# Attention and expert layers in one kernel: other places for two query loads, products of zeros ahead of the keys, another order of the value loads and means, and a ReLU in halves

## The reference

```python
# attention: a window of 16 either way, and 24 block summaries for all
k_sum = k.reshape(B, H, 24, 32, D).max(axis=3)
v_sum = v.reshape(B, H, 24, 32, D).mean(axis=3)
a = softmax([where(|i-j| < 16, scale*q@k.T, -1e9), scale*q@k_sum.T + log(32)])
attn = a @ concat([v, v_sum])
# first layer
h = x @ w_in
y = where(h > 0, h, exp(min(h, 0)) - 1) @ w_out
# second layer: the best expert of each token, times its gate
e = argmax(norm(y) @ norm(expert_emb).T / tau)
out = gate * (relu(y @ w1[e]) @ w2[e])
```

## Time and profile before

| what | value |
|---|---|
| median of 3 runs | 552.57 us (551.87 to 552.78) |
| the profiled execution's own time | 555.51 us |
| its span, first to last instruction | 553.8 us |
| TensorE busy, share of the span | 533.6 us, 96% |
| VectorE, ScalarE, GpSimd busy | 303.0, 234.3, 78.3 us |
| mean granted clock of TensorE | 0.992 of full |
| moved by DMA | 49.23 MB |

### The profile page before, as it was taken

How to read it: one execution, slowest core, us unless ns; L and a number is a source line. 1 busy time by engine, 2 the same in 40 slices (tenths; PEclk the granted TensorE clock), 3 DMA queues, 4 the chain that set the end, 5 groups by cost and what they waited for, 6 DMA issues and landing times.

```text
span 553.8 us, 11727 instructions
## 1 busy us (share of the span) xinstructions
PE 533.6 (96%) x3892; PEld 457.5 (83%) x3893; DVE 303.0 (55%) x672; ACT 234.3 (42%) x528; POOL 78.3 (14%) x210
## 2 busy tenths in 40 slices
PE   5898999999999999999999999999999999999995
PEld 4686888888888888888888899888778888888883
DVE  4667887544644465446642557667585265232552
ACT  5575664454544444444433245463072152121440
POOL 6300111010120000000000000110311222111221
PEclk9898999999999999999999999999999999999999
DMA  9999321323131112110100440010775156101000
GB/s 196 267 259 314 82 47 25 88 57 80 43 101 25 25 25 63 25 24 15 39 1 1 162 181 1 20 58 1 243 295 201 38 190 192 45 30 35 19 19 24
DMA packets 63499, 49.23 MB, mean 89 GB/s; under 512 B 46038, under 2 KB 52182, under 8 KB 63456
## 3 DMA queue, kind: packets, MB, share of 16 engines
q1 hardware_dynamic: 61056, 42.36, 26.7%
q0 software_dynamic: 2400, 6.30, 3.6%
HBM read 43.40 MB, written 6.82 MB: 91 GB/s over the span
## 4 chain that ended last, share of the span: by engine, by line
PE 93%; DVE 2%; DMA 2%; ACT 1%; issue 1%; SPq 1%; POOLq 0%; DVEq 0%; ACTq 0%
PE bank L932 24%; PE bank L974 8%; PE bank L981 8%; PE bank L987 8%; PE bank L1129 5%; PE bank L1171 5%; PE bank L1179 5%; PE bank L1137 5%; PE bank L1131 5%; PE bank L1173 5%; PE bank L910 2%; PE bank L892 2%; PE bank L1163 2%; PE bank L883 2%; DMA q_raw<-in_q 1%; PE bank L833 1%
## 5 line engine op out<-in xcount | busy, mean ns | idle before, releaser
L1324 ACT ACTIVATE el<-bank 128x512 f32<-128x512 f32 x48 | 28.7, 597 | 111.3 <-PE bank L932 110.0
L1605 DVE TENSOR_SCALAR el<-el 128x512 f32<-128x512 f32 x48 | 20.5, 427 | 90.2 <-ACT el L1324 90.2
L932 PE MATMUL bank<-x_hi,w_hi_parts 128*128 128x256 f32 x376 | 60.9, 283 | 0.0
L932 PE MATMUL bank<-x_hi,w_lo_parts 128*128 128x256 f32 x376 | 60.4, 282 | 0.0
L932 PE MATMUL bank<-x_lo,w_hi_parts 128*128 128x256 f32 x376 | 60.2, 282 | 0.0
L932 PEld LDWEIGHTS bank<-x_hi,w_hi_parts 128*128 128x128 f32 x376 | 53.6, 188 | 3.2 <-issue 0.2
L974 PE MATMUL bank<-w_hi_parts,g_hi 128*128 128x512 f32 x192 | 55.8, 413 | 0.0
L981 PE MATMUL bank<-w_lo_parts,g_hi 128*128 128x512 f32 x192 | 53.0, 398 | 0.0
L987 PE MATMUL bank<-w_hi_parts,g_lo 128*128 128x512 f32 x192 | 52.5, 395 | 0.0
L932 PEld LDWEIGHTS bank<-x_lo,w_hi_parts 128*128 128x128 f32 x376 | 51.5, 189 | 0.0
L932 PEld LDWEIGHTS bank<-x_hi,w_lo_parts 128*128 128x128 f32 x376 | 51.3, 188 | 0.0
(11 more groups left out here) (268 smaller groups left out, 909.5 us busy)
## 6 DMA issues: line engine op xcount, KB each, us to landing
raw<-in_moe_w SPq DMA_DIRECT2D x8, 2048.0 KB, 9.1
w_raw<-in_moe_w_in SPq DMA_DIRECT2D x8, 512.0 KB, 8.0
w_raw<-in_moe_w_out SPq DMA_DIRECT2D x8, 512.0 KB, 8.0
k_raw<-in_k SPq DMA_DIRECT2D x16, 192.0 KB, 3.2
v_raw<-in_v SPq DMA_DIRECT2D x8, 384.0 KB, 4.6
x_rows<-x SPq DMA_DIRECT2D x6, 512.0 KB, 3.0
q_raw<-in_q SPq DMA_DIRECT2D x44, 64.0 KB, 2.8
vwin<-in_v SPq DMA_DIRECT2D x32, 72.0 KB, 2.2
```

What stands on the lines that cost most here:

```text
L932: mm = pe.matmul(o, r32(w[:, at:at + P]), r32(x[i % 2][:, c, :]), start=(part == "hh" and c == 0), stop=(part == "lh" and c == DC - 1))
L1324: act.activation(el[n % 2], bank[:, H_BANK[n % 2], :], ACT.Exp).then_inc(e_act, 1)
```

## The change

- `load_q(4)` moves from behind `load_w_out(0)` to ahead of `load_w_in(1)`; `load_q(6)` moves from behind `load_w_out(3)` to behind `load_w_out(2)`, past in(4), windows 6 and out(3); `load_q(7)` moves from behind out(5) to behind out(3).
- The four value loads and the windows of pairs 0 to 3 are issued as values 0, 1, windows 0, values 2, 3, windows 1, 2, 3 in place of pair by pair.
- DVE sets `qT[1]` to zero first, and TensorE runs 11 products of these zeros ahead of the first keys and 4 more behind pair 0.
- The means of even pairs go to one PSUM bank, those of odd pairs to another, with other waits; `means(2)` stands ahead of `transpose_p(2)`. ACT copies out the means of pairs 0, 2 and 3 and DVE those of pair 1, where DVE had 0 and 1 and ACT 2 and 3.
- In the queues of ACT and DVE ahead of the first layer the order changes: `evacuate_p(3)` ahead of `split_high("in", 0)`, `store_x_high(3)` ahead of `split_high("in", 1)`, `split_low("in", 0)` behind all four `store_x_low`, and DVE's wait for the mask behind two key maxima.
- Slot 2 of the second layer makes its low products half by half and has its ReLU in two halves, as slot 0 had.

```diff
--- before.py
+++ after.py
@@ -368,8 +368,8 @@
         t_in, xs_t, xs_hi_v, xs_ev, h1_mm, h1_ev, h1_t, hT_hi_a, hT_ev = sems(
             "t_in xs_t xs_hi_v xs_ev h1_mm h1_ev h1_t hT_hi_a hT_ev")
-        h2_mm, g_cp, y_ev, t_cp, h1_half = sems(
-            "h2_mm g_cp y_ev t_cp h1_half")
+        h2_mm, g_cp, y_ev, t_cp, h1_half, zeros_ok = sems(
+            "h2_mm g_cp y_ev t_cp h1_half zeros_ok")
         def carry_waits(eng):
@@ -418,7 +418,7 @@
         def mean_bank(g):
-            return H_BANK[1] if g == 2 else ACC[0]
+            return ACC[0] if g % 2 else H_BANK[1]
         def turn_of(u):
             return u if u < PAIRS else u % 2
@@ -535,13 +535,18 @@
             for g in range(PAIRS):
                 load_k0(g)
                 load_q(g)
-            for g in range(PAIRS):
-                load_v0(g)
-                load_windows(g)
+            load_v0(0)
+            load_v0(1)
+            load_windows(0)
+            load_v0(2)
+            load_v0(3)
+            load_windows(1)
+            load_windows(2)
+            load_windows(3)
             load_w_in(0)
+            load_q(4)
             load_w_in(1)
             load_w_out(0)
-            load_q(4)
             load_w_in(2)
             load_windows(4)
             load_w_out(1)
@@ -549,16 +554,16 @@
             load_w_in(3)
             load_windows(5)
             load_w_out(2)
+            load_q(6)
             load_w_in(4)
             load_windows(6)
             load_w_out(3)
-            load_q(6)
+            load_q(7)
             load_w_in(5)
             load_windows(7)
             load_w_out(4)
             load_w_in(6)
             load_w_out(5)
-            load_q(7)
             load_w_in(7)
             load_w_out(6)
             load_w_out(7)
@@ -818,10 +823,10 @@
                 if batch == 0:
                     src, o = v_raw0[:, g, :], bank[KW:KC, mean_bank(g), g * P:(g + 1) * P]
                     pe.wait_ge(ld_v0[g], 16)
-                    if g == 2:
+                    if g == 0:
                         pe.wait_ge(k_ev, 2 * PAIRS)
-                    elif g == 3:
-                        pe.wait_ge(vs_ev, 2)
+                    elif g >= 2:
+                        pe.wait_ge(vs_ev, g - 1)
                 else:
                     src, o = v_raw1, bank[KW:KC, S_BANK[0], 0:P]
                     pe.wait_ge(v_two, g + 1)
@@ -1081,6 +1086,13 @@
                     if M_PLACES[g] == place:
                         means(g, 1)
+            def fill(n):
+                for _ in range(n):
+                    pe.matmul(bank[:, O_BANK, 0:P], qT[1][:, 0:P], qT[1][:, P:2 * P], start=True, stop=True)
+            pe.wait_ge(zeros_ok, 1)
+            fill(11)
             pe.wait_ge(ident_ok, 1)
             def keys_and_queries(g):
@@ -1089,6 +1101,7 @@
                 transpose_q(g)
             keys_and_queries(0)
+            fill(4)
             keys_and_queries(1)
             scores(0)
             keys_and_queries(2)
@@ -1102,8 +1115,8 @@
             means(1, 0)
             transpose_p(1)
             values(0)
+            means(2, 0)
             transpose_p(2)
-            means(2, 0)
             values(1)
             means(3, 0)
             transpose_p(3)
@@ -1154,7 +1167,11 @@
                     pe.wait_ge(raw_lo1, QUARTERS * run + (c + 1))
                     up_high(c, range(HALVES), base)
                 pe.wait_ge(xs_ev, s + 2)
-                up_low(range(HALVES), base).then_inc(h1_mm, 1)
+                if isinstance(s, int) and s == FILL:
+                    up_low((0,), base).then_inc(h1_half, 1)
+                    up_low((1,), base).then_inc(h1_mm, 1)
+                else:
+                    up_low(range(HALVES), base).then_inc(h1_mm, 1)
             def transpose_h(s):
                 pe.wait_ge(h1_ev, s + 2)
@@ -1283,8 +1300,13 @@
                          bank[KW:KC, S_BANK[0]:S_BANK[0] + 1, 0:P].to_broadcast([NSUM, WINS, P])
                          ).then_inc(vs_ev, 1)
-            def evacuate_last_means(g):
+            def evacuate_first_means(g):
                 act.wait_ge(m_mm, g + 1)
+                if g == 0:
+                    act.wait_ge(vw_zero, 1)
+                else:
+                    act.wait_ge(vs_ev, 2)
                 act.copy(vwin[KW:KC, g, :, :], means_of(g)).then_inc(vs_ev, 1)
             def exps(u):
@@ -1418,19 +1440,19 @@
             exps(1)
             evacuate_p(0)
             exps(2)
+            evacuate_first_means(0)
             evacuate_p(1)
             exps(3)
             store_x_high(0)
+            evacuate_first_means(2)
             evacuate_p(2)
-            act.wait_ge(vs_ev, 2)
-            evacuate_last_means(2)
+            evacuate_first_means(3)
+            evacuate_p(3)
             store_x_high(1)
-            evacuate_last_means(3)
             split_high("in", 0)
-            evacuate_p(3)
             store_x_high(2)
+            store_x_high(3)
             split_high("in", 1)
-            store_x_high(3)
             split_high("out", 0)
             behind(-5)
             for n in range(-1, NS - 1):
@@ -1484,10 +1506,15 @@
             roots(1)
             store_x2T(NB - 1, 0, O_BANK)
             store_x2T(NB - 1, 1, S_BANK[1])
-            act.wait_ge(h1_half, 1)
-            act.activation(h_sb[:, 0:512], bank[:, 0, :], ACT.Relu)
-            act.wait_ge(h1_mm, 1)
-            act.activation(h_sb[:, 512:F2], bank[:, 1, :], ACT.Relu).then_inc(h1_ev, 1)
+            def relu_halves(s):
+                act.wait_ge(h1_half, s // FILL + 1)
+                if s > 0:
+                    act.wait_ge(h1_t, 2 * s)
+                act.activation(h_sb[:, 0:512], bank[:, 0, :], ACT.Relu)
+                act.wait_ge(h1_mm, s + 1)
+                act.activation(h_sb[:, 512:F2], bank[:, 1, :], ACT.Relu).then_inc(h1_ev, 1)
+            relu_halves(0)
             hT_high(0)
             shifted_exps(1)
             relu(1)
@@ -1500,7 +1527,7 @@
             with act.If(there > 0):
                 high_w1(1)
                 high_w2(1)
-            relu(2)
+            relu_halves(FILL)
             there, run = starting_run(act, slice(3, 4))
             with act.If(there > 0):
                 high_w1(run())
@@ -1526,6 +1553,7 @@
                 ins.then_inc(dve_c, 1)
                 dve.wait_ge(dve_c, nch[0])
+            dve.memset(qT[1], 0.0).then_inc(zeros_ok, 1)
             dve.sem_inc(h2_mm, 1)
             dve.sem_inc(raw_lo1, 2 * QUARTERS)
             dve.sem_inc(raw_lo2, 2 * QUARTERS)
@@ -1558,10 +1586,10 @@
                 dve.tensor_reduce(kmaxT[:, g, :], kT[:, g, HALO:HALO + S].rearrange("p (n b) -> p n b", b=BLK),
                                   AX.X, ALU.max).then_inc(kmx, 1)
-            def evacuate_first_means(g):
+            def evacuate_second_means():
                 dve.wait_ge(m_mm, 2)
-                dve.wait_ge(vw_zero, 1)
-                dve.tensor_copy(vwin[KW:KC, g, :, :], means_of(g)).then_inc(vs_ev, 1)
+                dve.wait_ge(vs_ev, 1)
+                dve.tensor_copy(vwin[KW:KC, 1, :, :], means_of(1)).then_inc(vs_ev, 1)
             def softmax_max(u):
                 j = u // PAIRS
@@ -1793,9 +1821,9 @@
                     if K_PLACES[g][1] == place:
                         key_maxima(g, 1)
-            dve.wait_ge(mask_ok, 1)
             key_maxima(0, 0)
             key_maxima(1, 0)
+            dve.wait_ge(mask_ok, 1)
             softmax_max(0)
             key_maxima(2, 0)
             softmax_max(1)
@@ -1804,15 +1832,14 @@
             softmax_max(2)
             weights(1)
             softmax_max(3)
-            evacuate_first_means(0)
-            evacuate_first_means(1)
+            evacuate_second_means()
             weights(2)
             store_x_low(0)
             weights(3)
             store_x_low(1)
-            split_low("in", 0)
             store_x_low(2)
             store_x_low(3)
+            split_low("in", 0)
             split_low("in", 1)
             split_low("out", 0)
             for n in range(-1, NS - 1):
```

## The result

The changed kernel takes 548.81 us (median of 6, 548.42 to 549.35) against 552.67 us for the kernel before beside it (6 runs, 551.87 to 555.57). The ratio is 0.9921, with a 95% interval of 0.9895 to 0.9948: 3.9 us faster. The forecast was 546.8 us, 5.8 us faster, with a range of 545.0 to 550.3.

What follows compares the result with a forecast made beforehand. TensorE's own work bounds the kernel from about 50 us on; earlier gains carry to the end one for one. 3.8 + 1.7 + 0.4 - 0.1 = 5.8 us; 552.57 - 5.8 = 546.8 us, range 545.0 to 550.3.

Steps and rivals of the forecast that it cites:

- head start of 1.5 us: `project(0)` on TensorE begins at 35.6, 1.5 us sooner, held there by queries 5 landing and out(1)'s cast with `g_high(0)`.
- another landing of queries 5 as a sign of being wrong: The forecast is wrong if queries 5 or out(1) land at another time than now; queries 5 were put at 35.5.
- Queries 6: Queries of unit 6 turned on TensorE at 41.85 instead of 45.67, after a new wait of 0.3 us.
- 3.8 us for queries 6: Gain from turning the queries of unit 6 at 41.85 instead of 45.67 on TensorE.
- 1.7 us for the clock: Behind the wait for queries 6, the 4 us at granted clock 0.57 go: 1.7 us gained.
- the clock falls once, elsewhere: Rival: the lower clock comes near `project(0)` and `hidden(2)`, leaving 4.5 us of gain, 548.1 us; chance 0.28.
- the same wait, moved: Rival: TensorE stands at 41.55 as long as now and the clock falls; 1.9 us gained, 550.7 us; chance 0.12.
- The zeros: Products of zeros at the start: 0.2 us each, hidden in waits and costed at nothing; at most 0.8 us otherwise.
- reserve of 1.6 us: Slack of the early part before `project(0)`, covering a late clock rise, a late value window or 0.5 us more for zeros.
- ReLU: Second layer, slot 2: ACT's ReLU on the chain falls from 1.03 to 0.60 us, gaining 0.4 us.
- What is late next: Behind queries 6: 0.1 us waiting for out(1)'s low part at `project(1)`; out(3) later, nothing lost, reserve 0.9 us.
- The rule on loads: Skill page's 2.0 us plus bytes over 436 GB/s, 3.2 us for 512 KB; the trace showed 7.8 to 9.5 us.

Runs made afterwards that it cites:

- a3: The changed kernel with the three query loads back at their old places: 552.38 us against 552.07 for the kernel before.
- a2: The kernel before with only the three query loads at their new places: 550.59 us against 552.07 for the kernel before.
- b2: The kernel before with the new query load places and slot 2's ReLU in halves, old start: 550.00 us against 552.63 for the kernel before.
- c3: The changed kernel run again without edit: 548.88 us against 552.46 for the kernel before.
- b1: The kernel before with only slot 2's low products and ReLU in halves: 552.01 us against 552.63 for the kernel before.
- a1: The kernel before run again without edit: 552.52 us over 12 runs, against 552.07; its profiled execution took 551.86 us.
- c4: b3 with 7 zero products in place of 11 at the start: 548.61 us against 552.46 for the kernel before.
- c1: The changed kernel without its 15 products of zeros: 548.64 us against 552.46 for the kernel before.
- b4: b3 with queries 5 and 6 loaded one weight piece sooner still: 548.26 us against 552.63 for the kernel before.
- b3: The changed kernel with g_high(0) ahead of out(1)'s cast on ACT, queries 5's copy and g_high(1) ahead of out(2)'s: 547.72 us against 552.63 before.
- a4: The kernel before with 9 identity products on TensorE ahead of queries 6: 552.99 us against 552.07 for the kernel before.

## Why the prediction was right, and where it was off

**The mechanism held, the size did not.** Landings, and ACT's casts and copies behind them, decide when TensorE can go on between 28 and 42 us, and the place in SP's queue decides the landings: queries 6 landed at 44.2 in a3 and at 39.4 in the change, which differ in the places of the query loads only. a3 shows that the start without the queries gives nothing; a2 shows 1.5 us for the queries without it, and b2 2.6 us with the ReLU. The measured 548.81 lies outside the forecast's own range of 545.8 to 547.8; it lies in the wide one because that was drawn to take in the rivals.

**The head start of 1.5 us** was foreseen by two landings, queries 5 at 35.5 and the cast of out(1) with `g_high(0)` at 35.3. In the trace after TensorE stands for both, 0.38 us for queries 5 and then 0.56 for out(1), and `project(0)` begins at 34.91, in c3 at 35.7. But queries 5 landed 1.6 us sooner than I said, at 33.9 (34.8 in c3), and were not the last: out(1) with `g_high(0)`, which ended at 34.81, was. The prediction had named another landing of queries 5 as a sign of being wrong. It cost nothing here, as the limit by out(1) had been put only 0.2 us below it and held in its place; that `project(0)` came within 0.7 us owes something to luck. Half of the 1.5 us were the first trace's own, too: with the old start and a clock that did not fall from 22 to 28 us, b1 and b2 reach `project(0)` at 35.75 and 35.60, 0.7 to 0.8 us behind the changed kernel.

**Queries 6** were turned 0.6 us sooner than I said, and not for their landing: they had landed by 39.4. Of the two limits at nearly the same time, 41.85 for the landing and 41.95 for ACT's copy of queries 5, the second was the true one.

**The step that was mis-sized** is the terms of 3.8 us for queries 6 and 1.7 us for the clock, and the sentence behind the sum, that the distance of the profiled execution from the median "is nothing" for a difference of 6 us. That distance was 2.9 us, and the traces of before say what it was made of: the first trace reaches `project(2)` at 54.31 and that of a1 at 50.71, 3.6 us apart, and their spans differ by 3.7 us. From the trace of a1 to that of the change, queries 6 move by 43.62 - 41.29 = 2.3 us and the clock term is zero; with 0.4 for the ReLU the sum is 2.7 us. The two executions are 551.86 - 549.35 = 2.5 us apart, and the medians 3.9 and 3.6 in the two sessions that have the change, as many executions of before, by the estimate in a1, do fall to the lower clock once. Had the two terms been discounted for an execution 2.9 us above the median, the whole gain would have come to 5.8 - 2.9 = 2.9 us and the forecast to 549.7; the measured 3.9 us lie between the two.

**The rival "the clock falls once, elsewhere"** named the right time (548.1) for the wrong reason: no trace of the changed kernel shows a clock below 1.00 between 4 and 52 us. The gain is smaller because many executions of before lack one or both of their stretches at the lower clock, and not because the clock falls after the change. The rival "the same wait, moved" (550.7) was not seen.

**The zeros** cost more than the 0.2 us each that I took. The row of 2.46 us has twelve records, and these are six products, not twelve (the loop over `KT` = 6 in `means`; an fp32 product stands as two records), so the row says 0.41 us. Eleven zeros took 4.30 us and seven in c4 3.35 us, 0.48 each. They ended 0.7 us behind the landing of the first keys. It was hidden, as I had said that a reserve of 1.6 us would hide it, and c1 shows that with the new order they matter neither way.

**ReLU:** 0.4 us forecast; 0.7 us of waiting fell to 0.3.

**What is late next** was right in one place: out(3) did land late for ACT (0.76 us) and the reserve took it. The 0.1 us for the low part of out(1) was not needed. b4 shows that this reserve is thin: one query load more ahead of a weight piece, and the low parts are the wait (0.60 us).

**The rule on loads** ("DMA: Bandwidth & Descriptors" of the Trainium skill, section "Anatomy of one DMA — SWDGE (gpsimd) path", given there for the other kind of queue, with an estimate of 3.2 us for 512 KB) does not fit the trace after either: ACT began the cast of out(1) at 33.25 on its landing, 9.3 us behind an issue at 23.98.

## What to carry to other kernels

A wait for a load deep in a full DMA queue is no fixed number, here 1.1 to 3.1 us for the same code up to that place, and the lower clock came behind its long values only (2.61, 3.10 and 3.12 us, not 1.10). Before such a term goes into a sum, ask how far the profiled execution lies from the median; here it lay 2.9 us off, and most of that was in the terms being summed. A head start in front of a wait on a load is worth nothing until the load moves, and moving the load alone gave 1.5 us of the 3.9, so cost the two as one. When a load is moved ahead in a full queue, name who was using the reserve of the loads behind it; the first move was free here, and a second one gave nothing.

## What the runs showed of the hardware

- Products of 128 by 128 in fp32 stand as two records each (11 products, 22 records). At the higher clock they took 0.27 us each (4 in 1.06 us), and at the start of the span, from 1.3 us on, 0.48 and 0.46 (7 in 3.35 us in c4, 11 in 5.07 us in b3). The eleven in the change, 4.30 us or 0.39 each, lie between.
- Transposes did not keep the clock from rising. In the first trace of before TensorE ran nothing but transposes until 8.95, and the eight small score products (16 records) there already took 0.64 us, as they do later at a granted clock of 1.00; in a1, at 9.26, they took 1.08. In c1 the six transposes of the first keys took 1.51 us at 4.75 and those of the third pair 0.87 us at 9.89. The page "TensorE: Matmul & The Clock Gate" of the Trainium skill, section "Part 4: PE-mode transpose", says that the full clock does not engage for transpose mode; these rows disagree with it for fp32.

```profile
8.95 0.64 PE L883 MATMUL bank<-kb,qT 64*64 64x120 f32 x16
```

- The same load landed up to 2 us apart in different executions: queries 6, at their old place in the queue, at 43.5 (a4), 43.6 (a1), 44.7 (b1) and 45.6 us behind the same code, and at 44.2 behind the new start (a3).
